# Gated linear attention and two MLPs on one core: the attention from unit 1 on in chunks of 64 tokens instead of 128

## The reference

```python
batch, n_heads, seq, head_dim = (4, 8, 768, 48)        # n_tokens, d_model, d_ff = (3072, 384, 2048)
for t in range(S):
    state = alpha[:, :, t, :, None] * state + np.einsum('bhd,bhe->bhde', k[:, :, t], v[:, :, t])
    y[:, :, t] = np.einsum('bhd,bhde->bhe', q[:, :, t], state)
x = y.transpose(0, 2, 1, 3).reshape(B * S, H * D)
h = x @ w_in;  x = np.maximum(h, 0.0) ** 2 @ w_out     # first MLP
h = x @ w2_in; x = (h / (1.0 + np.exp(-h))) @ w2_out   # second MLP
```

## Time and profile before

| | |
|---|---|
| three runs | 898.69, 899.08, 900.78 us (median 899.08) |
| profiled execution | 901.13 us, its span 899.5 us |
| TensorE busy | 887.6 us (99%), 5050 matmul records |
| VectorE, ScalarE, GpSimd busy | 384.4 (43%), 398.5 (44%), 65.6 us (7%) |
| stretch with attention beside the first MLP | about 38 to 421 us |

### The profile page before, as it was taken

How to read it: one execution, slowest core, us unless ns; L and a number is a source line. 1 busy time by engine, 2 the same in 40 slices (tenths; PEclk the granted TensorE clock), 3 DMA queues, 4 the chain that set the end, 5 groups by cost and what they waited for, 6 DMA issues and landing times.

```text
span 899.5 us, 13308 instructions
## 1 busy us (share of the span) xinstructions
PE 887.6 (99%) x5050; PEld 732.8 (81%) x5050; DVE 384.4 (43%) x684; ACT 398.5 (44%) x726; POOL 65.6 (7%) x97
## 2 busy tenths in 40 slices
PE   7999999999999999999999999999999999999997
PEld 6788888888888888888888888888888888888897
DVE  7578866675556557662433312212212212212310
ACT  4765554445455445543756533233323233323520
POOL 2454200000000000000132000000000000000000
PEclk9999999999999999999999999999999999999999
DMA  9895443333333223311323200200101101100100
GB/s 158 225 241 116 97 116 74 73 71 104 85 78 100 65 65 75 91 24 45 122 89 106 71 1 0 71 1 19 52 0 36 36 1 35 36 1 1 36 11 28
DMA packets 106216, 59.76 MB, mean 66 GB/s; under 512 B 56416, under 2 KB 99808, under 8 KB 106144
## 3 DMA queue, kind: packets, MB, share of 16 engines
q1 hardware_dynamic: 100784, 51.84, 23.8%
q0 software_dynamic: 2048, 6.29, 2.2%
q10 hardware_dynamic: 3312, 0.69, 0.6%
HBM read 45.02 MB, written 9.44 MB: 61 GB/s over the span
## 4 chain that ended last, share of the span: by engine, by line
PE 98%; DMA 1%; ACT 0%; issue 0%; ACTq 0%; DVE 0%; DVEq 0%
PE h_ps L782 43%; PE z_ps L796 41%; PE job_ps L683 3%; PE job_ps L814 3%; PE job_ps L768 2%; PE job_ps L762 1%; PE job_ps L694 1%; PE job_ps L705 1%; PE z_ps L814 1%; PE h_ps L636 1%; DMA nat_q<-in_q 1%; PE z_ps L733 0%; PE z_ps L654 0%; PE z_ps L743 0%; PE z_ps L737 0%
## 5 line engine op out<-in xcount | busy, mean ns | idle before, releaser
L1231 DVE TENSOR_TENSOR g_lo<-g,g_hi 128x512 fp32r<-128x512 f32 x177 | 123.2, 696 | 373.9 <-ACT g_hi L994 243.0
L782 PE MATMUL h_ps<-x_hi,win_hi 128*128 128x512 f32 x576 | 224.7, 390 | 0.8 <-ACT g L991 0.8
L782 PE MATMUL h_ps<-x_hi,win_lo 128*128 128x512 f32 x576 | 224.1, 389 | 0.0
L782 PE MATMUL h_ps<-x_lo,win_hi 128*128 128x512 f32 x576 | 224.1, 389 | 0.0
L989 ACT ACTIVATE g<-h_ps 128x512 f32<-128x512 f32 x96 | 57.4, 598 | 232.1 <-PE h_ps L782 232.1
L991 ACT ACTIVATE g<-h_ps 128x512 f32<-128x512 f32 x96 | 57.3, 597 | 193.6 <-PE h_ps L782 193.6
L782 PEld LDWEIGHTS h_ps<-x_hi,win_hi 128*128 128x128 f32 x576 | 108.1, 188 | 23.8 <-POOL win_lo L575 1.2
L782 PEld LDWEIGHTS h_ps<-x_hi,win_lo 128*128 128x128 f32 x576 | 108.1, 188 | 22.5
L782 PEld LDWEIGHTS h_ps<-x_lo,win_hi 128*128 128x128 f32 x576 | 108.1, 188 | 22.2
L796 PE MATMUL z_ps<-g_hi,wout_hi 128*128 128x512 f32 x288 | 116.3, 404 | 0.0
L994 ACT ACTIVATE g_hi<-g 128x512 fp32r<-128x512 f32 x177 | 111.8, 632 | 5.7
(11 more groups left out here) (142 smaller groups left out, 818.2 us busy)
## 6 DMA issues: line engine op xcount, KB each, us to landing
z_scratch<-z_sb SPq DMA_DIRECT2D x18, 256.0 KB, 2.5
x_raw<-z_scratch SPq DMA_DIRECT2D x6, 768.0 KB, 4.5
v_sb<-in_v SPq DMA_DIRECT2D x44, 96.0 KB, 2.7
out_x<-z_sb SPq DMA_DIRECT2D x80, 48.0 KB, 1.7
nat_a<-in_alpha SPq DMA_DIRECT2D x40, 88.0 KB, 2.2
nat_k<-in_k SPq DMA_DIRECT2D x40, 88.0 KB, 2.5
nat_q<-in_q SPq DMA_DIRECT2D x40, 88.0 KB, 2.3
nat_a<-in_alpha SPq DMA_DIRECT2D x40, 80.0 KB, 2.2
```

Of the source, the lines that this page charges most:

```text
L782: last = nc.tensor.matmul(h_ps[f % 2][:], w[:, f, tile(kk)], x[par][:, kk, :], start=(kk == TILES[0] and n == 0), stop=(kk == TILES[-1] an ...
L1231: nc.vector.tensor_tensor(low, g[f % 2][:], high.bitcast(F32), ALU.subtract).then_inc(g_lo_made, 1)
```

## The change

Pairs from 4 on work in chunks of 64 tokens, two for each batch: scans, K and Q by halves of a unit (`HALVES` = 8 pieces of 64); the first chunk's whole product is applied to the state, then the second's.

- Scores: sixteen matmuls of 64x64 tokens (`s_halves`), head 0 and 1 by row half, first and second chunk by column half of the array, instead of eight of 128x128; for each batch and head 128 rows of 64 elements are masked instead of 128.
- Sums for the state: sixteen matmuls over 64 tokens (`i_halves`), by token half into two banks; now a stage I of its own, one step before Y for pair 4 and 8, beside S for pairs 5 to 7, and from 9 on in the step of S, behind the second product (for pairs 20 to 23 the first chunk's alone, eight matmuls; transposes and copies are made for them too).
- State: VectorE's `i_stage` waits for the outputs of the pair before, multiplies the old state by the first chunk's product, waits for the sums, adds the first sums, multiplies by the second chunk's product, adds the second sums (for pairs 4 to 19). The two states for the outputs lie in the free half of `score`.
- Outputs: sixteen matmuls of 64 tokens from the two states, sixteen of 64 tokens from v and the scores, into separate places of two banks that lie side by side (`y_ps`). ScalarE copies the one half of them into `y_sb`, VectorE adds the other (`y_stage`), and this addition raises `y_copied`.
- Steps: n = 4: I in 5, Y in 6; n = 5 to 7: I with S, Y one later; n = 8: I in 16, Y in 17; n >= 9: I with S. VectorE issues I and Y behind `low_g`, ahead of stage A.

The diff, cut to its core:

```diff
     if n < 2 * PAIRS:
-        return {"A": 1, "KQ": 3, "S": 4, "Y": 5}[kind] + 3 * (n - PAIRS)
+        return {"A": 1, "KQ": 3, "S": 4, "I": 4 + (n == PAIRS), "Y": 5 + (n == PAIRS)}[kind] + 3 * (n - PAIRS)
     if n == 2 * PAIRS:
-        return {"A": 13, "KQ": 14, "S": 15, "Y": 16}[kind]
-    return {"A": -21, "KQ": -19, "S": -18, "Y": -16}[kind] + 4 * n
+        return {"A": 13, "KQ": 14, "S": 15, "I": 16, "Y": 17}[kind]
+    return {"A": -21, "KQ": -19, "S": -18, "I": -18, "Y": -16}[kind] + 4 * n
...
 def behind(kind, n):
 
-    return kind == "S" and n in (PAIRS, 2 * PAIRS)
+
+    return kind == "S" and n in (PAIRS, 2 * PAIRS) or kind == "I" and n not in (PAIRS, 2 * PAIRS)
...
         first_y, middle_y, later_y = z_ps[1], z_ps[0], (job_ps[2], job_ps[0])
-
-        def i_bank(n):
-            return job_ps[0] if n < PAIRS else job_ps[1]
+        half_i = (job_ps[2], job_ps[1])
+
+        half_score = [x[:].rearrange("s b t -> s (b t)")[:, 0:BATCH * HALF] for x in score]
+        half_state = [x[0:ROWS].rearrange("s b t -> s (b t)")[:, BATCH * HALF:BATCH * (HALF + HD)] for x in score]
...
+                    return
                 for b in range(BATCH):
                     for h in (0, 1):
                         r = head_rows(h)
                         last = nc.tensor.matmul(job_ps[1 + h][:, tile(b)], kp[n % 2][r, tile(b)], qp[n % 2][r, tile(b)],
                                                 start=True, stop=True)
                 last.then_inc(s_made, 1)
-                if n >= PAIRS:
-                    t_stage(n)
+
+            def s_halves(n):
+
+                for b in range(BATCH):
+                    for half in (0, 1):
+                        cols = slice(b * P + half * HALF, b * P + (half + 1) * HALF)
+                        for h in (0, 1):
+                            r = head_rows(h)
+                            last = nc.tensor.matmul(job_ps[1 + h][half * HALF:(half + 1) * HALF, b * HALF:(b + 1) * HALF],
+                                                    kp[n % 2][r, cols], qp[n % 2][r, cols], start=True, stop=True,
+                                                    skip_group_check=True)
+                last.then_inc(s_made, 1)
...
+            def i_halves(n):
+
                 wait(pe, kt_copied, n + 1)
                 v_loaded(n)
-                if n >= PAIRS:
-                    wait(pe, masked, 2 * n + 1)
-
+
+                wait(pe, masked, 2 * (n + 1))
                 for b in range(BATCH):
                     for h, cols in ((0, slice(0, 64)), (1, head_rows(1))):
-                        last = nc.tensor.matmul(i_bank(n)[cols, b * HD:(b + 1) * HD], kp_t[:, b, cols],
+                        for half in (0, 1) if has_state(n) else (0,):
+                            tokens = slice(half * HALF, (half + 1) * HALF)
+                            last = nc.tensor.matmul(half_i[half][cols, b * HD:(b + 1) * HD], kp_t[tokens, b, cols],
+                                                    v_tile(n)[tokens, b, h, :], start=True, stop=True, skip_group_check=True)
+                last.then_inc(i_made, 1)
...
                 if n >= PAIRS:
                     y_halves(n)
-                    if has_state(n):
-                        i_stage(n)
                     return
...
                 wait(pe, decayed, n - PAIRS + 1)
 
-                if has_state(n):
-                    wait(pe, kt_copied, n + 1)
+                wait(pe, kt_copied, n + 1)
                 v_flat = v_tile(n).rearrange("t b h d -> t (b h d)")
-                places = [(half, h, 2 * half + odd, 64 - 16 * half) for odd in (0, 1) for half in (0, 1) for h in (0, 1)]
-
-                def to(half, h, b, cols):
-                    return later_y[h][64 * half:64 * half + cols, tile(b % 2)]
-                for half, h, b, cols in places:
-                    at = (p * BATCH + b) * 64
-                    nc.tensor.matmul(to(half, h, b, cols), flat_state[head_rows(h), at:at + cols], qp[n % 2][head_rows(h), tile(b)],
-                                     start=(b % 2 == 0), stop=False, skip_group_check=True)
-                for odd in (0, 1):
-                    for h in (0, 1):
-                        for half, b, cols in ((0, odd, 64), (1, 2 + odd, HD)):
-                            at = (2 * b + h) * HD
-                            last = nc.tensor.matmul(to(half, h, b, cols), v_flat[:, at:at + cols], score[h][:, b, :],
-                                                    start=False, stop=True, skip_group_check=True)
+
+                def to(bank, b, place):
+                    rows = slice(0, 64) if b < 2 else head_rows(1)
+                    return later_y[bank][rows, place * HALF:(place + 1) * HALF], 64 if b < 2 else HD
+                for half in (0, 1):
+                    for b in (0, 2, 1, 3):
+                        for h in (0, 1):
+                            out_cols, cols = to(h, b, 2 * (b % 2) + half)
+                            nc.tensor.matmul(out_cols, half_state[half][head_rows(h), b * HD:b * HD + cols],
+                                             qp[n % 2][head_rows(h), b * P + half * HALF:b * P + (half + 1) * HALF],
+                                             start=True, stop=True, skip_group_check=True)
+                for h in (0, 1):
+                    for b in (0, 2, 1, 3):
+                        for half in (0, 1):
+                            tokens, at = slice(half * HALF, (half + 1) * HALF), (2 * b + h) * HD
+                            out_cols, cols = to(half, b, BATCH + 2 * h + b % 2)
+                            last = nc.tensor.matmul(out_cols, v_flat[tokens, at:at + cols],
+                                                    half_score[h][tokens, b * HALF:(b + 1) * HALF],
+                                                    start=True, stop=True, skip_group_check=True)
                 last.then_inc(y_made, 1)
...
-                half = UT // 2
-                nc.scalar.activation(y_sb[n % 2][:, 0:half], later_y[0][0:ROWS, 0:half], ACT.Copy)
-                nc.scalar.activation(y_sb[n % 2][:, half:UT], later_y[1][0:ROWS, 0:half], ACT.Copy).then_inc(y_copied, 1)
+
+                nc.scalar.activation(y_sb[n % 2][:].rearrange("p (c k t) -> p k c t", c=BATCH, k=2),
+                                     y_ps[0:ROWS, :].rearrange("p (k x) -> p k x", k=2)[:, :, UT // 2:].rearrange(
+                                         "p k (c t) -> p k c t", c=BATCH), ACT.Copy).then_inc(within_copied, 1)
...
                 for kind, n in beside(F):
-                    if kind == "S" and has_state(n):
+                    if kind == "S":
                         kt_copy(n)
                     if kind == "Y":
                         y_copy(n)
...
-                    nc.vector.tensor_tensor_scan(out=rest[n % 2][:, b, P - 1::-1], data0=turned(n, b)[:, ::-1], data1=floor[:],
+                wait(dve, decayed, n - 1 - PAIRS)
+                if PAIRS <= n < PAIRS + 2:
+                    nc.vector.memset(half_rest[n % 2][:, :, HALF:], 1.0).then_inc(ends_set, 1)
+                for i, (alpha_t, back, _) in enumerate(pieces(n)):
+                    wait(dve, a_made, BATCH * n + (i + 1 if n == 0 else BATCH))
+                    size = P if n < PAIRS else HALF
+                    nc.vector.tensor_tensor_scan(out=back[:, size - 1::-1], data0=alpha_t[:, ::-1], data1=floor[:, 0:size],
                                                  initial=1.0, op0=ALU.mult, op1=ALU.max).then_inc(rest_made, 1)
...
-                    else:
-                        wait(dve, state_made, n - 2 * PAIRS + 1)
-                    p = n % PAIRS
-                    nc.vector.tensor_tensor(state[:, p, :, 0:HD], state[:, p, :, 0:HD],
-                                            rest[n % 2][:, :, 0:1].to_broadcast([ROWS, BATCH, HD]), ALU.mult).then_inc(decayed, 1)
...
             def a_grow(n):
                 wait(dve, inverse_made, n + 1)
-                for b in range(BATCH):
-                    nc.vector.tensor_tensor_scan(out=grown[n % 2][:, b, 1:], data0=turned(n, b), data1=floor[:],
-                                                 initial=grown[n % 2][:, b, 0:1], op0=ALU.mult, op1=ALU.max).then_inc(scanned, 1)
+                for alpha_t, _, up in pieces(n):
+                    size = P if n < PAIRS else HALF
+                    nc.vector.tensor_tensor_scan(out=up[:, 1:], data0=alpha_t, data1=floor[:, 0:size],
+                                                 initial=up[:, 0:1], op0=ALU.mult, op1=ALU.max).then_inc(scanned, 1)
...
+                if n >= PAIRS:
+                    wait(dve, causal_set, 1)
                 for h in (0, 1):
-                    nc.vector.tensor_tensor(score[h][:], job_ps[1 + h][:].rearrange("s (b t) -> s b t", b=BATCH),
-                                            causal[:].unsqueeze(1).to_broadcast([P, BATCH, P]), ALU.mult).then_inc(masked, 1)
-
-            def state_stage(n):
+                    if n >= PAIRS:
```

(73 more changed lines are left out.)

89 lines of the change are left out of this document (52 added, 37 removed).

## The result

The changed kernel takes **902.28 us** (median of 9 runs, 901.86 to 903.82) beside 899.55 for the kernel before (9 runs on the same chip): a ratio of 1.0031, interval 1.0021 to 1.0042. It is slower by 2.7 us (1.9 to 3.8 by the interval). I had said 0.6 faster, and had let rival 2 begin at 901.8.

A forecast was written before the change was run, and what follows sets the result against it. TensorE, busy 887.6 of 899.5 us, was taken to bound the kernel. From 899.08 us, 9.6 gained on TensorE and 9.0 of waits for VectorE, all before step 18, gave 898.5 us, range 892 to 907.

The forecast's parts named there:

- rival 2: VectorE's round in steps 4 to 17 longer than counted, by small scans or more slow operations: 904 us; chance 0.20.
- First outputs and what stands before them: TensorE at pair 4's outputs: VectorE ready at 8.75 against 8.1, a wait of 0.7 us.
- Edge of unit 1: Steps 15 to 18, around pair 8 and unit 1's first product: waits of 8.3 us less 0.64 of gain.
- Scores of pair 8: TensorE waits 1.45 us there for VectorE's addition of pair 7's outputs, which stands behind K, Q and g_lo.
- First product 16: Unit 1's first product on TensorE: waits 4.3 us for x, which comes from VectorE's addition of pair 7's outputs.
- Outputs of pair 8: Behind unit 1's edge: TensorE waits 1.9 us for VectorE, which needs 9.1 behind x_lo against TensorE's 7.2.
- Rival 4: TensorE's clock falls behind the 4 us wait at unit 1's edge, up to 2 us hidden: 901 us; chance 0.05.
- TensorE's gain: Pairs 4 to 19 cost 3.30 us for 3.94, 0.64 less each; pairs 20 to 23 0.6 more in all: 9.6 us.
- VectorE's round: VectorE's work per pair grows about 1.4 us; scans of 64 at 0.19 and 0.24 us, sixteen taking 3.4 for 2.8.
- Three late places: 1 us in a round is 3 us: First outputs, unit edge and pair 8's outputs each grow with VectorE's round: 1 us there moves the time about 3.
- Rival 3: TensorE's four parts don't give 0.058 us a round, no record stream being faster: 927 us; chance 0.06 with rival 5.
- rival 5: TensorE's parts run as now, only cut up, rounds of 0.11 us: as rival 3; chance 0.06 together with it.

The follow-up runs named there:

- e3: Changed kernel with GpSimd's 32 subtractions for the low parts of the first MLP's weights replaced by setting those parts to zero: 900.88 us, ratio 1.0002.
- e7: Changed kernel with unread matmuls on TensorE, six ahead of the scores of pair 8 and fifteen behind its transposes: 906.07 us, ratio 1.0064.
- e2: Changed kernel with sixteen unread matmuls on TensorE behind the transposes of pair 8, where it waited for unit 1's x: 903.36 us, ratio 1.0038.
- e4: Changed kernel with the forward scans of pairs 6 to 23 run over 8 tokens instead of 64: 901.12 us, ratio 1.0014.
- e1: Changed kernel with VectorE's addition of pair 7's outputs moved ahead of the K and Q work of pair 8: 898.3 us, ratio 0.9987.
- h8: New form from pair 8 on only; pairs 4 to 7 keep the form and steps of the kernel before: 894.74 us, ratio 0.9949.
- e8: Kernel before, with VectorE instead of ScalarE copying the second half of the outputs, where the changed kernel adds: 904.21 us, ratio 1.0052.

## Why the prediction was wrong, step by step

The mechanism was the forecast one: TensorE wins in every pair, VectorE takes it back in pairs 4 to 8, where its cover is gone, and most of that at the edge of unit 1. The balance of 9.6 against 9.0 came out on the other side. By the ledger the difference of 3.2 us between forecast (-0.6) and trace (+2.6) lies in these terms (2.3, 0.2 at the edge, 0.7 behind it):

- **First outputs and what stands before them: 2.3 us, the step that failed.** I gave pair 4's outputs a wait of 0.7 with the durations of the earlier trace rows, which are those of pair 8, when GpSimd is done. At pair 4 GpSimd is at work, and I allowed 0.4 for that in all, from one row. Measured: 1.7 at the outputs, 0.5 at the scores of pair 5, and 0.3 on the first product of step 4. The rest, 0.5, is 0.045 less gain in each of four pairs and 0.3 more in the steps of pair 4, 0.2 of it in step 4 (5.34 us, and 5.17 in e3). e3_pool_light shows what most of it was: without GpSimd's subtractions 1.9 of the 2.3 are gone, and the kernel takes as long as the one before (900.88 for 900.14). The trace of before had the answer; its product with k of pair 4:

```profile
45.51 1.36 DVE L1184 TENSOR_TENSOR kp<-kp,decay 112x512 f32<-112x512 f32 x1
```

- **Edge of unit 1: right in sum (7.9 for 7.7), wrong in its parts, so partly by luck.** Scores of pair 8: 1.6 for 1.45 (the walk's own 14.85 less 13.5 is 1.35). First product 16: 3.6 for 4.3. Outputs of pair 8: no wait, where I had 1.9, and sums of pair 8 none for 0.3. In their place stands the slow clock: step 16 lasted 7.6 us (118.82 to 126.44) and in e7 5.1 (119.84 to 124.94). Rival 4 had foreseen this, with up to 2 us hidden behind VectorE, though its "near double" set the transposes' 0.53 of the chain against a duration of 0.95; the duration at the full clock is 0.60 (start to start, step 16 gives 7.6 for 5.1). e7 and e2 show the exchange: at full clock the wait of 2.2 to 2.3 comes back.
- **TensorE's gain: forecast 0.7 us too high from step 20 on.** A pair gained 0.595, not 0.64. Scores, sums and outputs are each 0.01 to 0.02 longer than forecast (0.62, 0.84, 1.31 for 0.61, 0.82, 1.29). Late pairs cost 0.19 each for 0.14.
- **VectorE's round: right.** Scans of 64 in 1.57 and 2.05 us for eight, where I took 1.5 and 1.9; stage A 5.14 for 5.01; addition 0.68. The operations of stage I follow each other at 0.39 to 0.45 where I counted about 0.33, which is part of the 2.3.
- **"Three late places: 1 us in a round is 3 us" was wrong at the edge.** In e4 a stage 0.85 us shorter, at two of the three places, gave 1.0. At the edge TensorE waits for one chain of VectorE; of a wait that is shortened at the scores a part comes back at the next place (0.8 and 3.9 for 1.6 and 3.6). How a round's length acts at pair 4 was not tried alone.
- **Rival 3** (no stream of records under 25 ns apart), and with it rival 5, is out: 32 records of the scores in 0.62 us, entry included, are under 20 ns each. For records of different parts of the array the rule of the Trainium skill ("TensorE: Matmul & The Clock Gate", part 1) does not hold here; within one part 0.058 us is above it.

The chances: slower had 0.29, 0.20 of it rival 2. That rival named two ways. Small scans were not it (1.57 and 2.05 for 1.5 and 1.9); "more such slow operations" is what happened at pair 4, and I had priced it too low. The sign hung on little: without the failed step the trace would stand at +0.3, so the 0.7 of TensorE's gain went against the forecast as well.

## What to carry to other kernels

A change that makes the bound engine's work shorter and a covered engine's longer gains in every period and loses where the cover is thin; applied only where the cover stands (here from pair 9), it kept the gain (6.5 us at step 62, 5.8 at the end) and left out the loss (+0.4 at step 20 for the changed kernel's +8.8). When a walk through VectorE's order is made for one place, take the durations from that place, with what GpSimd does there. When an operation changes its engine, look at what stands ahead of it on the new one: moved behind K and Q, one copy of 0.4 us cost 2.8.

## What the runs showed of the hardware

- VectorE operations of 512 elements with two inputs in SBUF took 1.35 to 1.55 us beside a GpSimd subtraction in four places, and 0.69 alone or beside GpSimd's settings to zero (e3); in another place VectorE kept 0.67 and the subtraction took 1.63 for 1.01. The maskings, with one input in PSUM, kept 0.42.
- A wait of TensorE does not always bring the clock down. It fell to 0.50 behind the wait of 1.6 us at the scores of pair 8 (the changed kernel, e2), in the waits of 3.9 and 4.0 (e4, e3), and after waits of 1.7 (e1, e4) and 2.3 us (e7). It stayed at 1.00 after 1.7 at the same place in the changed kernel, 1.6 in h8, 2.3 in e1 and 2.6 in e8. Runs of one kernel differ too (mean clock 0.994 to 0.998 in e4, 0.997 to 1.000 in e8). What decides was not tried.
- At 0.50 a step of two products and the sums took 7.6 us for 5.1.
- A block of 32 small matmuls in four 64x64 parts costs about 0.14 to 0.16 us of entry and eight rounds of 0.058 (scores 0.62, sums 0.60; the outputs, 64 matmuls, 1.08). The product of 128x128 parts behind it is 0.23 to 0.24 longer; behind the scores' transposes it is 0.05.
- The stretch from the last matmul to the end of the span took 2.8 us in four traces and 4.5 to 4.9 in seven, and kernels that differ by one line lie on both sides (e3 and e4). Such a step can stand between two medians. Why there are two levels was not tried.
